# Routing each batch as its attention ends, top-1 tiles read from one DRAM region per expert, and a dense stage on expert-sorted rows

## The reference, cut to what matters

```python
# 1. attention, 4 batches x 8 heads, causal window of 128, ALiBi bias
attn = softmax(mask(q @ k.T / 8 + bias)) @ v           # -> x, 2304 x 512
# 2. top-1 mixture: each token goes through one of 8 experts
e = argmax(x @ w_gate);  g = softmax(x @ w_gate)[e]
y = g * (relu(x @ w1[e]) @ w2[e])                      # F = 1024
# 3. dense mixture: each token goes through all 4 experts
out = sum_e p[:, e] * (relu(y @ w1'[e]) @ w2'[e])      # p: domain_probs / their sum
```

## Time and profile before

| | us |
|---|---|
| three runs | 1350.09, 1348.51, 1344.07 (median 1348.51) |
| the profiled execution | 1346.97, of which the span of instructions is 1344.8 |
| PE busy | 1269.1 (94%) |
| DVE, ACT, POOL busy | 552.6, 274.4, 354.6 |
| mean granted clock of PE | 0.967 |

### The profile page before, as it was taken

How to read it: one execution, slowest core, us unless ns; L and a number is a source line. 1 busy time by engine, 2 the same in 40 slices (tenths; PEclk the granted TensorE clock), 3 DMA queues, 4 the chain that set the end, 5 groups by cost and what they waited for, 6 DMA issues and landing times.

```text
span 1344.8 us, 20902 instructions
## 1 busy us (share of the span) xinstructions
PE 1269.1 (94%) x6800; PEld 1125.3 (84%) x6801; DVE 552.6 (41%) x1195; ACT 274.4 (20%) x574; POOL 354.6 (26%) x180
## 2 busy tenths in 40 slices
PE   6999991399999996999999999999999999999999
PEld 5888881388888885899999999999999999999997
DVE  7656646122232322444444444444444444444444
ACT  4555640011111212411111111111111111111110
POOL 4444414465657753310300300300300300300000
PEclk9999985699999997999999999999999999999999
DMA  6476614687878873210300300300300300100003
GB/s 221 172 251 215 245 53 163 223 309 279 318 291 325 330 287 115 63 63 0 125 0 0 125 0 0 125 0 0 125 0 0 125 0 0 63 0 0 0 24 117
DMA packets 37450, 159.86 MB, mean 119 GB/s; under 512 B 6560, under 2 KB 6560, under 8 KB 23072
## 3 DMA queue, kind: packets, MB, share of 16 engines
q1 hardware_dynamic: 21504, 88.48, 18.0%
q0 software_dynamic: 9856, 59.77, 12.4%
q10 hardware_dynamic: 6048, 11.01, 2.4%
HBM read 135.14 MB, written 24.12 MB: 118 GB/s over the span
## 4 chain that ended last, share of the span: by engine, by line
PE 93%; POOL 2%; issue 2%; DMA 2%; DVE 1%; ACT 0%; ACTq 0%; DVEq 0%; POOLq 0%
PE ps L1167 30%; PE ps L1180 29%; PE ps L1118 9%; PE ps L1104 8%; PE ps L1029 6%; PE ps L1012 3%; PE ps L1000 2%; POOL x_sorted L455 2%; PE ps L1001 1%; PE ps L1129 1%; PE ps L1051 1%; DMA x_rows<-x_sorted 1%; PE ps L1083 1%; PE ps L1043 1%; POOL y_gathered L523 0%
## 5 line engine op out<-in xcount | busy, mean ns | idle before, releaser
L1167 PE MATMUL ps<-x_t_hi,w_split 128*128 (+1 forms) x1536 | 392.1, 336 | 0.0
L1180 PE MATMUL ps<-w_split,h_t_hi 128*128 128x512 f32 x1152 | 356.9, 391 | 0.0
L1167 PEld LDWEIGHTS ps<-x_t_hi,w_split 128*128 128x128 f32 x1536 | 280.3, 188 | 7.5 <-issue 0.2
L950 DVE SCALAR_TENSOR_TENSOR out_sums<-ps,domain_share,out_sums 128x512 f32 (+1 forms) x270 | 202.8, 751 | 164.8 <-PE ps L1180 164.8
L1167 PE MATMUL ps<-x_t_lo,w_split 128*128 (+1 forms) x768 | 258.1, 336 | 0.0
L1180 PEld LDWEIGHTS ps<-w_split,h_t_hi 128*128 128x128 f32 x1152 | 214.6, 188 | 41.2
L647 ACT ACTIVATE h_t_hi<-ps 128x384 fp32r<-128x384 f32 x192 | 94.5, 492 | 687.3 <-PE ps L1167 687.3
L936 DVE SCALAR_TENSOR_TENSOR h_t_lo<-ps,h_t_hi 128x384 fp32r<-128x384 f32 x192 | 107.1, 558 | 300.4 <-ACT h_t_hi L647 300.4
L446 POOL TENSOR_TENSOR w_split<-w_raw,w_split 128x2048 fp32r<-128x2048 f32 x44 | 202.4, 4610 | 103.5 <-DMA w_split<-weights 77.5
L1180 PE MATMUL ps<-w_split,h_t_lo 128*128 128x512 f32 x576 | 226.0, 392 | 0.0
L440 POOL DMA_DIRECT2D w_split<-weights x20 | 11.0, 553 | 514.3 <-PE ps L1180 500.1
(11 more groups left out here) (130 smaller groups left out, 1002.4 us busy)
## 6 DMA issues: line engine op xcount, KB each, us to landing
w_split<-weights POOLq DMA_DIRECT2D x48, 1024.0 KB, 7.8
w_raw<-weights SPq DMA_DIRECT2D x48, 1024.0 KB, 5.1
qk_raw<-q_k_turned SPq DMA_DIRECT2D x16, 1152.0 KB, 7.7
x_sorted<-zeros SPq DMA_DIRECT2D x7, 1024.0 KB, 5.2
x_rows<-x_sorted ACTq DMA_DIRECT2D x21, 256.0 KB, 4.7
y_sorted<-y ACTq DMA_DIRECT2D x21, 256.0 KB, 4.4
v_one<-v_ones SPq DMA_DIRECT2D x16, 325.0 KB, 3.0
out<-out_sums SPq DMA_DIRECT2D x5, 768.0 KB, 3.6
```

What stands on the lines that cost most here:

```text
L950: v.scalar_tensor_tensor(out=a_, in0=ps[:, 2 + k, :], scalar=p_, in1=a_, op0=ALU.mult, op1=ALU.add).then_inc(acc_done, 1)
L1167: last = mm(ps[:, f, 0:GROUP], wt[:, q // 2, at:at + P], xt[:, c, x], start=(k == 0), stop=(k == 3 * DC - 1))
L1180: last = mm(ps[:, 2 + t, :], ht[:, par, f, t * P:(t + 1) * P], wt[:, 2 + q // 2, at:at + D], start=(k == 0), stop=(k == n - 1))
```

## The change

1. *x and its rows.* x has eight more columns (XW = 520): four for the token's domain share times its gate weight, one for the token's number, three unused. DVE writes each head's result straight into x; the copy by ACT is gone.
2. *Routing by batch.* The loop over batches is written out. Ten to twenty duos after a batch's last duo DVE runs, a step or two per duo, the chain shift, pick, mark, gate_sum, gate_share, read_ranks, count, add_ranks, put on 5 row blocks; PE makes the batch's ranks (rank, in a free part of PSUM bank 7), ACT its exponentials. The place of a token is its expert's region (of 2304 rows) plus the rows that the expert has so far, so it needs no later batch. POOL scatters batches 0, 1 and 2 after its splits for pairs 9, 13 and 15, and waits for each scatter to land. The last batch's chain and scatter stand after attention.
3. *Zeros.* Only the first 128 rows of each region are zeroed, at the start (8 DMAs); the rest of a region's tail is never read, since an expert's last tile is the last 128 of its rows and overlaps the one before.
4. *Tables.* They come after the last batch's places, on one partition: 41 DVE instructions in all. Two new ones give each tile's row in x and in y (where rows stand by expert without gaps).
5. *Top-1.* Loads and stores take their row from the tables. For each tile ACT also issues a copy, DRAM to DRAM, of the eight extra columns (128 rows of 32 bytes, move_aux).
6. *Dense.* It works on 18 blocks of 128 sorted rows. ACT loads six blocks during the last top-1 tile and the rest as buffers come free; PE turns blocks 0 and 1 before the last down, and blocks 2 to 5 after it. The scaling by the gate is gone. The y of the last tile is stored after that, since it is read only with the last blocks.
7. *Store.* POOL scatters 18 blocks of out_sums to their tokens with indirect DMAs as the last quarter finishes them.

```diff
+        SCATTER_AFTER = {2 * PAIRS + 1: 0, 3 * PAIRS + 1: 1, NP - 1: 2}
...
+            for n in range(1, NP):
+                split_qk(n, n % 2)
+                if n in HI_AFTER:
+                    i = HI_AFTER[n]
+                    g.dma_start(Wh[0][:, TOP1_ORDER[i], :], weights[:, i * CHUNK:(i + 1) * CHUNK]).then_inc(hi_in[i], 16)
+                if n in SCATTER_AFTER:
+                    scatter(SCATTER_AFTER[n])
+                    pool.wait_ge(scattered, 16 * QT * (SCATTER_AFTER[n] + 1))
+            scatter(B - 1)
...
+            ROUTE = {1: shift, 2: pick, 3: mark, 4: gate_sum, 5: gate_share, 7: count, 8: add_ranks, 9: put}
...
+            def move_aux(i):
+                at, to = x_row(i), y_row(i)
+                act.wait_ge(aux_moved, (i + 1) * 16)
+                act.dma_start(ys_dram[bass.ds(to, P), D:XW], xs_dram[bass.ds(at, P), D:XW]).then_inc(aux_moved, 16)
...
+                else:
+                    act.wait_ge(y_stored, total * 16 - 16)
+                    act.wait_ge(aux_moved, total * 16 + 16)
+                    for r in range(YG):
+                        load_y(r)
...
-            for r in range(RT):
-                n = ROWS[r % QT]
-                if r >= YG:
-                    pool.wait_ge(g_turned, r - YG + 1)
-                g.indirect_dma_start(yg_sb[0:n, r % YG, :], None, ys_dram,
-                                     bass.IndirectOffsetOnAxis(ap=place_u[0:n, r:r + 1], axis=0)).then_inc(gathered[r % YG], 16)
...
+            for k in range(TOK):
+
+                pool.wait_ge(acc_done, GT * last + GT + (k + 1))
+                g.indirect_dma_start(out, bass.IndirectOffsetOnAxis(ap=token[:, k:k + 1], axis=0),
+                                     acc[:, k, :], None).then_inc(stored, 16)
...
             tile(total - 1, False, False)
+            turn_y([0, 1])
             down(total - 1)
...
+            act.wait_ge(tiles_done, total + 1)
+
+            def high_rows(rs):
 
                 for r in rs:
                     act.wait_ge(g_turned, r + 1)
+                    a.copy(x2h[:, :, r * P:(r + 1) * P],
+                           ps[:, turn_bank(r), :].rearrange("p (c t) -> p c t", c=DC)).then_inc(g_hi, 1)
+                    if r + YG < TOK:
+                        if r + YG == TOK - 2:
+                            act.wait_ge(y_stored, total * 16 + 16)
+                        act.wait_ge(g_kept, r + 1)
+                        load_y(r + YG)
...
             low_rows(rows_of_group(0))
+            copy_y(total - 1)
             low_rows(rows_of_group(1))
...
-            turn_y(rows_of_group(0))
+            turn_y([2])
             pe.wait_ge(split_done, E1 * CHUNKS + 2)
             turn_y(rows_of_group(1))
             up2_first(0)
```

More of the change, by code:

```diff
@@ L271, in rows_of_group, with pair_due, batch_due, head_due @@
         def rows_of_group(g):
-            return [r for r in range(RT) if column(r) // GROUP == g]
-        def column(r):
-            return r // QT * S + r % QT * P
+            return range(g * GT, (g + 1) * GT)
         def tiles_total(eng):
             return eng.value_load(tab_x[:], min_val=0, max_val=E1 - 1) + N // P
[L282 to L298, removed]
+        def pair_due(j, lag):
+            n = (j - lag) // QT
+            return [n] if (j - lag) % QT == 0 and 0 <= n < NP else []
+        def batch_due(j, after):
+            at = j - (QT * (PAIRS - 1) + PV_LAG + 10) - after
+            b = at // (QT * PAIRS)
+            return [b] if at % (QT * PAIRS) == 0 and 0 <= b < B else []
+        def head_due(j):
+            return [h for h in range(HEADS) if (h * QT + QT - 1) // 2 + PV_LAG + 1 == j]
         @block.sync
@@ new lines, in _ @@
+            last = B - 1
+            shift(last)
+            pick(last)
+            mark(last)
+            gate_sum(last)
+            gate_share(last)
+            read_ranks(last)
+            count(last)
+            add_ranks(last)
+            put(last)
+            cnt_, til_, end_, cend_, cst_, rest_, some, upto, next_, ends = (t8[:, i, :] for i in range(10))
+            e_row, i_row = iota8[0:1, :], iota_t[0:1, :]
+            by_tile = lambda ap: ap.unsqueeze(1).broadcast_to([1, TILES, E1])
@@ new lines, in turn_x @@
+            def turn_x(n):
+                b, hp = n // PAIRS, n % PAIRS
+                pe.wait_ge(heads_normed, n * 2 + 4)
+                pe.wait_ge(xpair_copied, n + 1)
+                if hp == 0:
+                    pe.wait_ge(logits_summed, b + 1)
+                if hp == 1 and b > 0:
+                    pe.wait_ge(ranks_read, b)
+                for t in range(QT):
+                    o = ps[:, 6, t * P:(t + 1) * P] if t < 4 else ps[:, 7, 160:160 + 64]
+                    ins = turn(o, x_sb[0:ROWS[t], b * QT + t, hp * P:(hp + 1) * P], ident[0:ROWS[t], 0:ROWS[t]])
+                ins.then_inc(xpair_turned, 1)
```

741 lines of the change are left out of this document (374 added, 367 removed).

## The result

| | kernel before | changed kernel |
|---|---|---|
| median of the runs, us | 1347.25 | 1388.41 (1387.12 to 1390.66) |
| ratio to before | | 1.031 [1.028, 1.034] |
| profiled execution, us | 1346.97 | 1387.12 |
| its span, us | 1344.8 | 1385.5 |
| mean granted clock of PE | 0.967 | 0.949 |

The forecast was 1322 us with a range up to 1332. The changed kernel is 3% slower. The rest of this text cuts both spans at the same events and takes the difference piece by piece.

A forecast was written before the change was run, and what follows sets the result against it. PE was taken as the bound, busy 1269.1 of 1344.8 us, with 59 us idle in two stretches that the change aims at. Terms summed to -24.8: span 1320.0, execution 1322 us, range 1312 to 1332.

The follow-up runs named there:

- e3: The kernel before with its last three 256 KB stores of out_sums issued by POOL instead of SP, as plain DMAs: 1353.0 us, ratio 1.0033.
- e2: The kernel before with only the v load moved ahead of the q and k load in SP's loop: 1401.4 us, ratio 1.037.
- e12 to e14: Changed kernel with load order, routing steps and scatters mended, tiles shifted by 1536, 1152 and 768 bytes; one profiled execution each, spans 1328.7, 1335.5 and 1334.9 us.

## What to carry to other kernels

When a loop on a DMA queue is written anew, compare it line by line with the old: which wait stands ahead of which load, and how much time each load has between issue and use in the profile. A load that is moved behind one late semaphore can cost most of its landing time at every turn (4.6 us in the mean here), and where PE stalls for it, its clock as well. Price a small operation from rows where the same neighbours are busy, not from rows where they are idle; and try mends in combination too, since either half alone showed nothing here.

## What the hardware showed that I had not expected

- A shift of the tiles by 640 or 1152 bytes slows the dense matmuls from 391 to 394 ns (about 5 us in all), a shift by 768, 1024 or 1536 doesn't.
- POOL's closing drain takes 8.3 us from its last store (7.8 in e3, where the stores are plain; 14.0 in the kernel before, off the path), DVE's 0.8 and SP's 0.01. In this kernel the last DMA is better issued by SP than by POOL.
- A 40-column operation of DVE on SBUF operands can last until the end of the POOL operation beside it: 2.62, 2.18 or 0.95 us instead of 0.20, by how much of POOL's was left.
- A stall of PE costs again in its clock: 23.4 us of waiting in attention came with 38.9 us more busy time at a clock of 0.81; in e2, with no instruction added, 23.0 us with 36.0 at 0.83.
- In e12 to e14 DVE stood 3 to 8 us beside the late scatters for a cause that the profile calls "remote"; this stays open.
